# Gathered rows of a mixture-of-experts stage are transposed through DRAM and VectorE instead of TensorE

## The reference

```
x  = retention(q, k, v)            # 2 x 8 heads x 768 x 64, decayed running state
h  = relu(x @ w_in); g = sigmoid(conv3(h)); x2 = (h * g) @ w_out      # 512 -> 1024 -> 512
for each token s of each batch:                                         # 8 experts
    fresh = argmax(x2[s] @ w_gate)
    e = fresh if s == 0 or sigmoid(x2[s] @ w_local) < 0.5 else e of token s-1
    out[s] = p[e] * (relu(x2[s] @ w1[e]) @ w2[e])       # 512 -> 1024 -> 512
```

## Time and profile before

| what | value |
|---|---|
| median of three executions | 419.17 us (419.12 to 419.39) |
| the profiled execution | 419.02 us |
| its span in the trace | 416.9 us |
| TensorE matmul busy | 405.5 us (97%) |
| VectorE, ScalarE, GpSimd busy | 228.8, 209.7, 105.1 us |
| share of TensorE in the chain that ended last | 92% |

### The profile page before, as it was taken

The page is one execution under the profiler, slowest core; times in us unless marked ns, Lnnn a source line. Parts: engine busy times, 40 slices in busy tenths (PEclk is TensorE's granted clock), DMA queues, the critical chain, the costliest instruction groups (busy, mean ns, idle before and its releaser), DMA issues.

```text
span 416.9 us, 7057 instructions
## 1 busy us (share of the span) xinstructions
PE 405.5 (97%) x2597; PEld 342.1 (82%) x2598; DVE 228.8 (55%) x293; ACT 209.7 (50%) x293; POOL 105.1 (25%) x104
## 2 busy tenths in 40 slices
PE   7999999999999999999999999999999999999992
PEld 3888799887889987879788888888888888888881
DVE  4788739973004879477376511106961273655640
ACT  2334678670214865380557423327852563747640
POOL 3344873000000000026622212213232222322320
PEclk9999999999999999999999999999999999999998
DMA  8999900000520007753474711015691173572500
GB/s 291 406 412 415 396 6 2 0 2 0 201 91 12 2 0 314 292 192 109 169 290 150 328 50 50 26 50 201 269 416 54 44 307 155 181 291 64 222 17 25
DMA packets 16152, 67.74 MB, mean 162 GB/s; under 512 B 2623, under 2 KB 4159, under 8 KB 11776
## 3 DMA queue, kind: packets, MB, share of 16 engines
q1 hardware_dynamic: 12928, 58.87, 35.9%
q0 software_dynamic: 2912, 8.13, 5.7%
q10 hardware_dynamic: 288, 0.41, 0.3%
HBM read 58.49 MB, written 10.22 MB: 165 GB/s over the span
## 4 chain that ended last, share of the span: by engine, by line
PE 92%; DMA 5%; SPq 1%; ACT 1%; issue 0%; POOL 0%; DVE 0%; POOLq 0%; ACTq 0%
PE ps L996 26%; PE ps L998 25%; PE ps L997 25%; DMA kv<-qkv 5%; PE ps L1262 4%; PE ps L1236 2%; PE ps L1047 2%; PE ps L1044 2%; PE ps L1026 1%; PE ps L1093 1%; PE ps L1010 1%; PE ps L1072 0%; PE ps L1168 0%; PE ps L1102 0%; PE ps L1159 0%
## 5 line engine op out<-in xcount | busy, mean ns | idle before, releaser
L929 DVE TENSOR_TENSOR hT<-ps,hT 128x512 fp32r<-128x512 f32 x34 | 23.5, 691 | 88.5 <-ACT hT L643 88.5
L916 DVE TENSOR_TENSOR wx<-raw_w,wx 128x1024 fp32r<-128x1024 f32 x56 | 65.1, 1218 | 2.8 <-ACT wx L584 1.6
L996 PE MATMUL ps<-wx,hT 128*128 128x512 f32 x136 | 56.1, 413 | 0.3 <-issue 0.3
L584 ACT CAST wx<-raw_w 128x1024 fp32r<-128x1024 f32 x56 | 55.0, 1049 | 0.0
L996 PE MATMUL ps<-wx,xT 128*128 128x512 f32 x136 | 54.7, 402 | 0.2 <-DVE xT L952 0.2
L998 PE MATMUL ps<-wx,xT 128*128 128x512 f32 x136 | 53.2, 391 | 0.0
L998 PE MATMUL ps<-wx,hT 128*128 128x512 f32 x136 | 53.1, 391 | 0.0
L997 PE MATMUL ps<-wx,xT 128*128 128x512 f32 x136 | 53.0, 390 | 0.0
L997 PE MATMUL ps<-wx,hT 128*128 128x512 f32 x136 | 53.0, 390 | 0.0
L996 PE MATMUL ps<-x,win 128*128 128x384 f32 x128 | 43.2, 337 | 0.0
L998 PE MATMUL ps<-x,win 128*128 128x384 f32 x128 | 42.8, 334 | 0.0
(11 more groups left out here) (162 smaller groups left out, 760.0 us busy)
## 6 DMA issues: line engine op xcount, KB each, us to landing
raw_w<-w_exp SPq DMA_DIRECT2D x28, 1024.0 KB, 4.7
qk<-qkv SPq DMA_DIRECT2D x7, 768.0 KB, 9.7
raw_first<-w_exp SPq DMA_DIRECT2D x4, 1024.0 KB, 8.0
kv<-qkv SPq DMA_DIRECT2D x4, 768.0 KB, 11.5
x_rows<-x2n SPq DMA_DIRECT2D x11, 256.0 KB, 2.8
kv<-qkv SPq DMA_DIRECT2D x7, 384.0 KB, 10.2
x_early<-x2n SPq DMA_DIRECT2D x10, 256.0 KB, 2.3
win_raw<-w_in SPq DMA_DIRECT2D x4, 512.0 KB, 12.2
```

Of the source, the lines that this page charges most:

```text
L584: nc.scalar.copy(wx[:, slot, 0, c], raw).then_inc(wx_hi[w], 1)
L916: nc.vector.tensor_tensor(wx[:, slot, 1, c], raw, wx[:, slot, 0, c].bitcast(F32), ALU.subtract).then_inc(w2_lo_dve if w else w1_lo_dve, 1)
L929: nc.vector.tensor_tensor(lo, psHT[:, 512 * a:512 * a + 512], hi.bitcast(F32), ALU.subtract).then_inc(hT_done, 1)
L996: mm(o, lh, rl, start=first, stop=False)
```

## The change

TensorE no longer turns the gathered rows in steps 1 to 16. SyncE stores `xg` into a DRAM tensor `x_block` and loads it back in four quarters into `xq`, so that the 32 x 32 blocks stand on the partitions where they must end, and VectorE transposes the blocks of `xq` into `xF` with one instruction of 128 x 512. ScalarE and VectorE make the high and the low part from `xF` instead of from PSUM. The rows of w1 are put in another order on the host (`quarters`), to fit. The first two row sets (steps 0 and 1) are still turned by TensorE, in the new layout: by matmuls with 32 columns of `xg` as the stationary operand, 16 in place of 4 transposes. The last 128 rows of x2 are computed and stored in halves made of four strips of 64 columns each.

The step's order changes too: in ScalarE's and VectorE's programs the pass over x comes behind both halves of h, and waits there for VectorE's transpose; the weight pieces stay behind the whole of it. In TensorE's program both `turn_h` are moved inside a group of `three`, ahead of its last matmul. SyncE's program now goes step by step: the store and the four loads of a step, and behind the first ones of an expert its weight loads. GpSimd's gather waits for the store to have landed, and no longer for TensorE.

The diff, cut to what the argument speaks of:

```diff
@@ -392,14 +402,36 @@
                 sp.wait_ge(w1_lo_dve, 4 * e - 5)
                 raw(0, e, raw_w1[s], raw_w1_in[s])
 
-            with sp.Fori(2, E - 2, 2) as ee:
-                raw_w2_next(ee)
-                raw_w1_next(ee + 1, 1)
-                raw_w2_next(ee + 1)
-                raw_w1_next(ee + 2, 0)
-            raw_w2_next(E - 2)
-            raw_w1_next(E - 1, 1)
-            raw_w2_next(E - 1)
+            def step(g):
+
+                sp.wait_ge(gathered, 16 * g + 32)
+                sp.wait_ge(x_turned, 16 * g + 32)
+                sp.dma_start(x_block, xg[:]).then_inc(x_stored, 16)
+                sp.wait_ge(x_stored, 16 * g)
+                for q in range(NQ):
+                    sp.dma_start(xq[TR * q:TR * q + TR],
+                                 x_block[:, P * q:P * q + P].rearrange("(b j) n -> j b n", j=TR)
+                                 ).then_inc(quartered, 16)
+
+            def expert(e, s, ahead):
+
+                first, end = block_range(sp, e)
+                if not (isinstance(e, int) and e == 0):
+                    step(first)
+                    if ahead > 0:
+                        raw_w2_next(e + 1)
+                    if ahead > 1:
+                        raw_w1_next(e + 2, s)
+                rest(sp, first, end, step)
+
+            sp.wait_ge(tables, 1)
+            expert(0, 0, 2)
+            with sp.Fori(1, E - 3, 2) as ee:
+                expert(ee, 1, 2)
+                expert(ee + 1, 0, 2)
+            expert(E - 3, 1, 2)
+            expert(E - 2, 0, 1)
+            expert(E - 1, 1, 0)
 
 
         @block.gpsimd
...
@@ -467,7 +498,7 @@
             def step(g):
 
                 scatter_before(g)
-                pool.wait_ge(gathered, 16 * g + 32)
+                pool.wait_ge(x_stored, 16 * g)
                 gather(g + 2)
 
             def wide(a):
...
@@ -632,10 +664,9 @@
                 nc.scalar.activation(hs[:, 512 * a:512 * a + 512], psP1[:, 512 * a:512 * a + 512],
                                      ACT.Relu).then_inc(h_done, 1)
 
-            def x_hi(g):
-
-                act.wait_ge(xg_free, g + 2)
-                nc.scalar.copy(xT[:, 0].rearrange("p k t -> p (k t)"), psXT).then_inc(xT_hi, 1)
+            def x_hi(g, source):
+
+                nc.scalar.copy(xT[:, 0].rearrange("p k t -> p (k t)"), source).then_inc(xT_hi, 1)
 
             def h_hi(g, a):
 
...
@@ -666,13 +698,14 @@
                     weights_hi(0, e, slot, (3,))
                 h_hi(g, 0)
                 relu(g, 1)
-                x_hi(g + 1)
                 h_hi(g, 1)
+                act.wait_ge(x_turned, 16 * g + 48)
+                x_hi(g + 1, xF[:].rearrange("p k t -> p (k t)"))
 
             for n in range(2):
                 act.wait_ge(x2_done, TT + n)
-                h = slice(DM // 2 * n, DM // 2 * n + DM // 2)
-                nc.scalar.copy(x2n[:, (TT - 1) % 3, h], psXh[n]).then_inc(x2_out, 1)
+                nc.scalar.copy(column_half(x2n[:, (TT - 1) % 3, :], n),
+                               psXh[n].rearrange("t (q c) -> t q c", q=NQ)).then_inc(x2_out, 1)
                 act.wait_ge(x_first, n + 1)
                 nc.scalar.copy(xT[:, 0, 2 * n:2 * n + 2], psX0[:, 2 * n:2 * n + 2]).then_inc(x0_hi if n == 0 else xT_hi, 1)
             act.wait_ge(tables, 1)
...
@@ -916,9 +951,15 @@
                     nc.vector.tensor_tensor(wx[:, slot, 1, c], raw, wx[:, slot, 0, c].bitcast(F32),
                                             ALU.subtract).then_inc(w2_lo_dve if w else w1_lo_dve, 1)
 
-            def x_lo(g):
+            def turn_x(g, waited):
+
+                dve.wait_ge(quartered, waited)
+                nc.vector.transpose(xF[:].rearrange("p k (q t) -> p k q t", q=NQ),
+                                    xq[:].rearrange("p q (k i) -> p k q i", k=KD)).then_inc(x_turned, 16)
+
+            def x_lo(g, source):
                 dve.wait_ge(xT_hi, g + 1)
-                nc.vector.tensor_tensor(xT[:, 1].rearrange("p k t -> p (k t)"), psXT,
+                nc.vector.tensor_tensor(xT[:, 1].rearrange("p k t -> p (k t)"), source,
                                         xT[:, 0].rearrange("p k t -> p (k t)").bitcast(F32),
                                         ALU.subtract).then_inc(xT_done, 1)
 
...
@@ -932,16 +973,18 @@
             def step(g):
 
                 h_lo(g, 0)
-                x_lo(g + 1)
                 h_lo(g, 1)
+                turn_x(g + 1, 64 * g)
+                x_lo(g + 1, xF[:].rearrange("p k t -> p (k t)"))
 
             def first_step(g, e, slot):
 
                 h_lo(g, 0)
                 if e is not None:
                     weights_lo(0, e, slot, (3,))
-                x_lo(g + 1)
                 h_lo(g, 1)
+                turn_x(g + 1, 64 * g)
+                x_lo(g + 1, xF[:].rearrange("p k t -> p (k t)"))
 
             dve.wait_ge(tables, 1)
             weights_lo(0, 0, 0, (0, 1, 2))
...
@@ -1112,8 +1157,8 @@
 
             def x2_half(n, k):
                 ts = slice(S - P, S)
-                ws = slice(DM * k + DM // 2 * n, DM * k + DM // 2 * n + DM // 2)
-                last = three(psXh[n], hg[:, 0, k, ts], hg[:, 1, k, ts], wout[:, 0, ws], wout[:, 1, ws],
+                wh, wl = (column_half(wout[:, w, DM * k:DM * k + DM], n) for w in range(2))
+                last = three(psXh[n].rearrange("t (q c) -> t q c", q=NQ), hg[:, 0, k, ts], hg[:, 1, k, ts], wh, wl,
                              k == 0, k == KF - 1)
                 if k == KF - 1:
                     last.then_inc(x2_done, 1)
...
@@ -1175,7 +1221,9 @@
                 pe.wait_ge(gathered, 16)
                 pe.wait_ge(x2_out, TT - 1)
                 for k in range(KD):
-                    last = nc.tensor.transpose(psX0[:, k, :], xg[:, P * k:P * k + P], ident)
+                    for q in range(NQ):
+                        last = mm(psX0[TR * q:TR * q + TR, k, :], xg[:, P * q + TR * k:P * q + TR * k + TR], ident,
+                                  start=True, stop=True)
                 last.then_inc(xg_free, 1)
 
             gate_first()
...
@@ -1262,37 +1312,38 @@
                     last = nc.tensor.transpose(psHT[:, P * k:P * k + P], hs[:, P * k:P * k + P], ident)
                 last.then_inc(ht_tr, 1)
 
-            def w1_part(a, k, slot):
+            def w1_part(a, k, slot, amid=None):
 
                 c = slice(FF * k + 512 * a, FF * k + 512 * a + 512)
                 o = psP1[:, 512 * a:512 * a + 512]
                 last = three(o, xT[:, 0, k, :], xT[:, 1, k, :], wx[:, slot, 0, c], wx[:, slot, 1, c],
-                             k == 0, k == KD - 1)
+                             k == 0, k == KD - 1, amid)
                 if k == KD - 1:
                     last.then_inc(p1_done, 1)
 
-            def w2_part(k, slot):
+            def w2_part(k, slot, amid=None):
 
                 c = slice(FF * KD + DM * k, FF * KD + DM * k + DM)
                 last = three(psO, hT[:, 0, k, :], hT[:, 1, k, :], wx[:, slot, 0, c], wx[:, slot, 1, c],
-                             k == 0, k == KF - 1)
+                             k == 0, k == KF - 1, amid)
                 if k == KF - 1:
                     last.then_inc(p2_done, 1)
 
-            def second_layer(g, e, slot):
+            def second_layer(g, e, slot, early):
 
                 pe.wait_ge(o_done, g + 1)
                 pe.wait_ge(hT_done, 2 * g + 1)
                 pe.wait_ge(w2_lo_dve, 4 * e + 2)
                 w2_part(0, slot)
-                turn_h(g, 1)
+                if early:
+                    turn_h(g, 1)
                 for k in range(1, KF):
                     if k == 4:
                         pe.wait_ge(hT_done, 2 * g + 2)
                         pe.wait_ge(w2_lo_dve, 4 * e + 3)
                     if k == 6:
                         pe.wait_ge(w2_lo_dve, 4 * e + 4)
-                    w2_part(k, slot)
+                    w2_part(k, slot, (lambda: turn_h(g, 1)) if k == 1 and not early else None)
 
             def step(g, e, slot):
 
...
@@ -1302,12 +1353,10 @@
                 for k in range(KD):
                     w1_part(0, k, slot)
                 w1_part(1, 0, slot)
-                w1_part(1, 1, slot)
-                turn_h(g, 0)
+                w1_part(1, 1, slot, lambda: turn_h(g, 0))
                 w1_part(1, 2, slot)
                 w1_part(1, 3, slot)
-                turn_x(g + 1)
-                second_layer(g, e, slot)
+                second_layer(g, e, slot, False)
 
             pe.wait_ge(x2_out, TT - 3)
             for k in range(KF):
...
@@ -1376,7 +1429,7 @@
         "w_out_t": tiles(inputs["moe_w_out"].T).reshape(P, KD, FF),
         "w_gl": tiles(np.pad(np.concatenate([inputs["moe2_w_gate"], inputs["moe2_w_local"]], axis=1),
                              ((0, 0), (0, WG - E - 1)))).reshape(P, KD, WG),
-        "w_exp": np.stack([np.stack([tiles(a), tiles(b)], axis=1)
+        "w_exp": np.stack([np.stack([quarters(a), tiles(b)], axis=1)
```

(14 more changed lines are left out.)

30 lines of the change are left out of this document (21 added, 9 removed).

## The result

The changed kernel takes 424.06 us (median of four, 423.02 to 424.44), the kernel before on the same chip 419.14 (418.5 to 419.39): 1.0116 times as long, 95% interval 1.0094 to 1.0137. It is slower by 4.9 us, where I had forecast 0.9. The profiled execution took 423.02 us; its span is 3.6 us longer than that of before.

The account below looks back on a forecast made before the run. TensorE, with 92% of the chain that ended last, was taken as the bound. - 7.12 + 1.6 + 6.0 + 0.55 = + 1.0 us on 419.02 gave 420.0, with the median 0.15 above it 420.1 us; range 416.2 to 424.5.

Parts of the forecast that it names:

- A: Experts' steps: TensorE's turn of xg leaves 16 steps at 0.445 us each, 7.12 us less.
- B: Turn_h inside a group of three: TensorE loses 0.06 us waiting for hT at 26 places, 1.6 us more.
- T + 1.95: In a step, VectorE ends the low part of hT 1.95 us after T, the start of a turn_h.
- C: Experts' borders: delayed weight pieces make ScalarE's relu late, 0.68 us at five and 2.58 at the one-block one, 6.0 more.
- D: The start: first_rows and step 1's turn by 16 narrow matmuls, 0.85 us a turn, together 0.55 us more.
- the rival of 431 us: Turns at the start: the narrow matmuls run one by one, 11.3 us more; chance 0.03.
- last_rows costs as before: Last rows of x2, stored in 256-byte strips: their TensorE work was forecast to add nothing.
- The way through DRAM: Store and reload of x: some 6.5 us, hidden, with 5 us free, under 2 behind the one-block expert.
- the x rows come late: Round trip 3 us longer: steps lose 0.5 us, one-block border 2; with slower transposes 424.0 us; late rows or slow transposes 0.20.

Follow-up runs that it names:

- a2: The changed kernel with both turn_h one matmul earlier, behind the first matmul of the group of three: 421.9 us, ratio 1.0069.
- b1: The kernel before with TensorE's turn of the gathered rows left out of steps 1 to 16 (stale rows): 417.81 us, ratio 0.9973.
- a1: The changed kernel with ScalarE's and VectorE's pass over x back ahead of the second half of h: 430.4 us, ratio 1.0265.
- a6: a1 with w1 loads behind an expert's last step, and VectorE's transpose ahead of its weight piece in an expert's first step: 419.76 us.
- a7: a6 with both turn_h one matmul earlier, as in a2: 419.3 us, ratio 1.0015.
- a8: The changed kernel with only SyncE's w1 loads moved, behind an expert's last step in place of its first: 424.87 us, ratio 1.0154.
- a5: The changed kernel with an extra VectorE transpose of 128 x 384 into unused tiles ahead of the real one in 16 steps: 426.45 us.
- a3: The changed kernel with a1's order of the x pass and a2's earlier turn_h together: 427.86 us, ratio 1.0200.
- a10: a3 with the transpose ahead of VectorE's weight piece and raw weights of experts 2 to 7 issued on ScalarE's queue: 428.34 us.
- a9: a7 with each w1 loaded one expert earlier and SyncE's loop over the experts written out: 424.55 us, ratio 1.0144.
- a11: The changed kernel with only the raw weights of experts 2 to 7 issued on ScalarE's queue: 428.23 us, ratio 1.0215.

## Why the forecast was right, and where it was off

**The turn removed (A), right as work.** No group on xg is left in the steps, and an undisturbed step is 11.82 us (a2). What stands in its place is told in b1: most of it was cover.

**Turn_h inside a group (B), right at its two places, and 1 us short beside them.** Forecast were 0.06 us at each place of hT. From 268.85 to 269.38 pass 0.53 us in place of two pitches (0.46): 0.07. The second place loses 0.05 (272.13 to 272.64). That is 0.12 a step, as forecast, and VectorE's low part of hT ends at T + 1.94 there, forecast T + 1.95. But the intervals give 12.00 - 11.82 = 0.18 a step, some 3.0 us over 16 steps with rounding, where the sum had 1.6: it took 26 places, since it left six to C (0.4), and it had no term for the remaining 0.06 a step (1.0). These lie in hundredths between other matmuls: the 27 pitches ahead of a turn_h take 6.15 us here and 6.12 in a2. Why, no run shows; a2 took them off together with the waits. The plain step was forecast at 11.8 to 12.0.

**The pass over x behind both halves (C), right.** Count from T = 282.30, the second turn_h: the transpose starts at T + 1.86 (284.16), the cast at T + 2.60 and the pieces at T + 3.12 (285.42), where the forecast had T + 1.87, T + 2.60 and T + 3.10. Over a plain step of 12.00 us the intervals lose 1.22, 0.36, 3.27, 0.69, 0.68 and 0.69 at the six borders, each with the step behind it but the second, whose next interval is already the one-block expert's. That is 6.9 us; forecast were 6.0. The clean five-piece borders agree with the 0.68 of the sum within 0.01 (over a plain step, which holds B, the sum's figure is 0.62, so a few hundredths of this are luck). The first border holds 0.47 of late quarters. Of the 3.27, 0.33 belong to the five-piece border ahead (its second turn_h at 3.61 in place of 3.28), which so costs 0.69 too; the one-block border costs 2.94 in place of 2.58. There seven pieces and five differ by 1.98 us from start to start, where the sum had subtracted lengths (1.90), and the gap of 0.27 us stood ahead of the evacuation: 0.69 + 1.98 + 0.27 = 2.94. a1, a6 and a7 nearly free the five-piece borders by the order (a8 shows that the loads alone don't), and a5 lengthens four of them. That makes the chain shown, not argued. The Trainium skill ("Vector Engine (DVE) Microarchitecture Reference", reshape front-end) stands well here: the estimate by its one element per cycle and lane, with the fixed part that the forecast added, was 0.69 us, and the trace has 0.70 to 0.71.

**The start (D), too small.** A turn by narrow matmuls takes 0.90 us (195.69 to 196.59), forecast 0.85, and they do run four at a time, so the rival of 431 us is out. But the start cost 1.47 in place of 0.55. The step that failed is "last_rows costs as before". Its three blocks of matmuls with `oh` take 0.99, 0.58 and 0.58 us from their start to the next matmul, where they took 0.82, 0.36 and 0.36, and another 0.18 us lie ahead of the last two: 0.8 in all. The turn of first_rows costs 0.47 more, and 0.09 ahead of it (195.48 to 195.69 where the pitch was 0.12); the turn in step 1 costs 0.19 more, forecast 0.11; the rest of the start is 0.1 shorter. The store in 256-byte strips landed later (the gather was issued at 203.11, has 201.88), but TensorE waited for nothing there, as forecast.

**The way through DRAM, hidden as forecast.** The store lands in 2.0 us, the loads issue in 1.75 (four of 0.44, where I had 0.35), and the quarters were late at two of 16 steps, by 0.47 and 0.30 us. The rival "the x rows come late" explains at most 0.5 us of after. Its price was 424.0, nearly what came, but its cause wasn't there: the agreement is luck. It became true when the transpose was moved ahead (a1, a3, a10), and when more weights were put in front of a store (a9). That cover had been worth more than it looked: C's late place for the transpose is what kept the trip hidden.

**The sum.** - 7.12 + 3.0 + 6.9 + 1.5 = + 4.3 us, less the 0.37 ahead at the start: + 3.9, against + 3.6 in the spans and + 4.0 between the profiled executions. The medians are 4.9 apart. The other 0.9 us lies between the profiled execution, the fastest, and the rest (423.9 to 424.44). The mean granted clock was 0.997 in the profiled execution and 0.990 to 0.995 in the others, and in other kernels longer waits at the one-block border cost 1 to 2 us by the clock, so that may be it; but no trace of a slower execution of after exists, and this stays open.

The forecast was 420.1 us with a range of 416.2 to 424.5, slower at 0.49: direction, mechanism and range held, the direction by little (420.1 against a bound of 420.0) and the range near its upper end. The middle was 4 us too low. For the profiled execution it was 3.0: B 1.4, D 0.9 and C 0.9, less the 0.37 at the start. The other 0.9 are the open part.

## What to carry to other kernels

Work taken off the bounding engine is worth only what the next chain leaves of it: here leaving the turn out altogether gave 1.0 of 7.1 us, and one such run would price a change before anyone writes it. A link added ahead of a long row of background work on an in-order engine costs its length wherever that row had no idle time behind it; look for the borders, and not for the plain step alone. And if the fix is an earlier place for the same link, check what its late place was hiding, since here a trip through DRAM came into the open.

## What the runs showed of the hardware

- A wait of TensorE could cost more than its length. Behind the waits of 2.90 and 3.73 us in a1, 2.95 in a7, 3.03 in a11, 3.06 in a2, 3.31 in a8, 3.49 in a3, 3.77 and 3.43 in a10, 4.09 and 2.63 in a9 the granted clock fell to the 1.2 GHz level for some microseconds (means of 0.50 to 0.78 over 3 to 8 us); behind 2.29 in the kernel after, 2.35 in a5 and 2.59 in a3 it stayed at 1.00. A fall added 1.6 to 3.1 us in a1 and a7. The wait's length alone doesn't set the price: 3.73 us cost 1.8 more, and 2.90 cost 3.1.
- 16 float32 matmuls with 32 stationary columns each took 0.90 to 0.99 us in place of 0.43 to 0.82 for the full-width ones that they replaced, and 8 of them 0.58 in place of 0.36; the start of the first came 0.07 to 0.09 us later behind a full-width matmul.
- A 256 KB store with 4 MB of weights ahead in its queue let its reload go 10.75 us after its issue (a9), against 2.0 us from issue to landing in the median of the stores in the kernel after.
- VectorE's transpose of 128 x 512 float32 in 32 x 32 blocks takes 0.70 to 0.71 us, as long as a subtraction of that shape (0.69).
